# Seven products in place of eight for the second layer's up projection, in the last six pairs of token blocks

## What is computed

```python
def _moe2_ref(x, w_in, w_out, g_ln):        # x: 3072 x 512, w_in: 512 x 1024, w_out: 1024 x 512
    h = x @ w_in
    e = np.exp(h - np.max(h, axis=-1, keepdims=True))
    sm = e / (np.sum(e, axis=-1, keepdims=True) + 1e-09)
    solu = h * sm
    mu = np.mean(solu, axis=-1, keepdims=True)
    var = np.mean((solu - mu) ** 2, axis=-1, keepdims=True)
    ln = (solu - mu) / np.sqrt(var + 1e-06) * g_ln
    return (ln @ w_out).astype(np.float32)
```

## Time and profile before

| | us |
|---|---|
| median of 3 runs (lowest, highest) | 970.91 (968.33, 972.44) |
| the profiled execution's own time | 976.88 |
| its span from the first to the last instruction | 975.1 |
| TensorE matmuls busy | 944.7 (97%), 5334 matmuls |
| VectorE, ScalarE, GpSimd busy | 644.2 (66%), 521.7 (54%), 136.4 (14%) |
| mean granted TensorE clock | 0.989 |

### The profile page before, as it was taken

How to read it: one execution, slowest core, us unless ns; L and a number is a source line. 1 busy time by engine, 2 the same in 40 slices (tenths; PEclk the granted TensorE clock), 3 DMA queues, 4 the chain that set the end, 5 groups by cost and what they waited for, 6 DMA issues and landing times.

```text
span 975.1 us, 14652 instructions
## 1 busy us (share of the span) xinstructions
PE 944.7 (97%) x5334; PEld 834.8 (86%) x5334; DVE 644.2 (66%) x1065; ACT 521.7 (54%) x911; POOL 136.4 (14%) x170
## 2 busy tenths in 40 slices
PE   8979999999999999999999999999999999999996
PEld 4666787787899999999999999999888888888875
DVE  3677895786778754454679877777375766666651
ACT  3554644554556433342546554555477866666641
POOL 4313301101115430000053101010100000000000
PEclk9799999999999999999999999999999999999998
DMA  9656545626153423131364616340510054351533
GB/s 271 194 168 201 171 165 164 194 114 189 48 215 115 157 80 121 50 127 52 131 226 146 235 57 232 111 166 25 179 57 32 20 143 91 94 128 46 110 85 86
DMA packets 103847, 126.61 MB, mean 130 GB/s; under 512 B 8160, under 2 KB 84320, under 8 KB 103776
## 3 DMA queue, kind: packets, MB, share of 16 engines
q1 hardware_dynamic: 98320, 109.28, 36.5%
q0 software_dynamic: 4736, 15.73, 4.7%
q10 hardware_dynamic: 720, 0.66, 0.2%
HBM read 77.41 MB, written 37.75 MB: 118 GB/s over the span
## 4 chain that ended last, share of the span: by engine, by line
PE 81%; DVE 7%; DMA 3%; issue 3%; ACT 2%; SPq 2%; POOL 0%; DVEq 0%; ACTq 0%; POOLq 0%
PE psum L949 11%; PE psum L952 11%; PE psum L951 11%; PE psum L385 7%; PE psum L386 7%; PE psum L387 7%; PE psum L985 6%; PE psum L987 6%; PE psum L988 6%; PE psum L842 3%; PE psum L876 3%; PE psum L866 2%; PE psum L855 2%; SPq L690 1%; DMA out<-out_buf 1%
## 5 line engine op out<-in xcount | busy, mean ns | idle before, releaser
L949 PE MATMUL psum<-xo_hi,w_hi 128*128 128x384 f32 x560 | 194.8, 348 | 6.5 <-DVE psum L1658 2.5
L951 PE MATMUL psum<-xo_lo,w_hi 128*128 128x384 f32 x560 | 187.9, 336 | 0.0
L952 PE MATMUL psum<-xo_hi,w_lo 128*128 128x384 f32 x560 | 187.9, 336 | 0.0
L949 PEld LDWEIGHTS psum<-xo_hi,w_hi 128*128 128x128 f32 x560 | 105.7, 189 | 12.7 <-DVE c L1662 4.4
L951 PEld LDWEIGHTS psum<-xo_lo,w_hi 128*128 128x128 f32 x560 | 105.7, 189 | 0.8 <-issue 0.3
L952 PEld LDWEIGHTS psum<-xo_hi,w_lo 128*128 128x128 f32 x560 | 105.4, 188 | 0.0
L1163 ACT ACTIVATE xo_hi<-b 128x768 fp32r<-128x768 f32 x84 | 70.7, 846 | 63.2 <-PE psum L988 52.4
L1538 DVE TENSOR_TENSOR xo_lo<-b,xo_hi 128x768 fp32r<-128x768 f32 x84 | 81.3, 970 | 34.6 <-ACT xo_hi L1163 34.4
L385 PE MATMUL psum<-w_in_hi,x_hi 128*128 128x512 f32 x192 | 75.9, 395 | 2.0 <-ACT h_buf L1284 2.0
L1658 DVE TENSOR_TENSOR psum<-psum,p_buf 128x384 f32<-128x384 f32 x48 | 27.1, 565 | 76.0 <-PE psum L952 76.0
L385 PE MATMUL psum<-w_out_hi,ln_t_hi 128*128 128x512 f32 x192 | 75.1, 391 | 1.2 <-DVE ln_t_lo L1775 1.2
(11 more groups left out here) (142 smaller groups left out, 2030.2 us busy)
## 6 DMA issues: line engine op xcount, KB each, us to landing
act_dram<-act_buf SPq DMA_DIRECT2D x48, 384.0 KB, 2.4
b<-act_dram SPq DMA_DIRECT2D x48, 384.0 KB, 4.8
ln_t<-z SPq DMA_DIRECT2D x80, 128.0 KB, 3.1
kq_buf<-k_t SPq DMA_DIRECT2D x32, 192.0 KB, 2.7
kq_buf<-q_t SPq DMA_DIRECT2D x64, 96.0 KB, 3.0
q_dec<-q_t SPq DMA_DIRECT2D x32, 192.0 KB, 2.5
w_raw<-weights POOLq DMA_DIRECT2D x12, 512.0 KB, 5.1
x_dram<-x_tile SPq DMA_DIRECT2D x4, 1536.0 KB, 6.0
```

Of the source, the lines that this page charges most:

```text
L949: pe.matmul(dst, hi[:, cols], xo_hi[:, i, kc, :], start=i in (P1, P7) and kc == 0, stop=False, skip_group_check=True)
L951: pe.matmul(dst, hi[:, cols], xo_lo[:, i, kc, :], start=False, stop=False, skip_group_check=True)
L952: mm = pe.matmul(dst, lo[:, cols], xo_hi[:, i, kc, :], start=False, stop=kc == HK - 1, skip_group_check=True)
```

## The change

The up projection of pairs 6 to 11 (blocks 12 to 23) is computed by seven products. A pair is a 2 x 2 block problem: two blocks of tokens by two halves of the 512 input features, times two halves of the input features by two halves of the 1024 outputs. Each product is 2 chunks by 3 matmuls of 512 columns, so a pair has 42 matmuls for its up where it had 48. In the even step TensorE does P1, P7, P6, P2, P5 (30 matmuls) and then `down2`, in the odd step P3, P4 (12 matmuls) and then `down2`. Sums of products accumulate in PSUM with copies in between: ScalarE copies P1's bank into another (`copy_xy`) and P7 out (`copy_p7`), VectorE adds twice (`add_u3`, `add_c22`), ScalarE copies three of the four quarters out (`copy_up`).

The four sums of the weights (8 pieces of 128 x 512) are made by GpSimd in stage D at t = 1 between its stores, and each is stored to DRAM before the next is made. In stage C GpSimd loads them back, and ScalarE and VectorE split them (`t_high`, `t_low`): pieces 0 to 3 in tile 0, 4 to 7 in steps (1, 0) and (1, 1). The four sums of the tokens are made for each pair by GpSimd (`make_s`), and the seven operands of 2 x 128 columns are split in three instructions on each engine (`s_high`, `s_low`; 512, 256 and 1024 columns).

Memory: `z` has one buffer in place of two, `x2_raw` is loaded for one pair at a time (`load_up`), `squares` takes the place of `d_squares`.

The core of the diff: GpSimd's sums of weights, TensorE's products and their order, ScalarE's order in a pair of steps, the wait ahead of the transpose, VectorE's order.

```diff
+        UP_ORDER = (P1, P7, P6, P2, P5, P3, P4)
+            def sum_t(p, a, at):
...
+                    pool.wait_ge(t_summed, at)
+                    pool.wait_ge(t_stored, DMA * at)
+                pool.tensor_tensor(t_sum[:], first, second, ALU.subtract).then_inc(t_summed, 1)
+                pool.wait_ge(t_summed, at + 1)
+                pool.dma_start(t_store(T_PIECES.index((p, a))), t_sum[:]).then_inc(t_stored, DMA)
             for t in range(B):
+                sum_some(t, 0, 4)
                 for q in range(2):
                     store_x2(t, q, 0, q, c11_copied, q)
+                sum_some(t, 4, 6)
                 for q in range(2):
                     store_x2(t, 2 + q, 1, 2 + q, c22_summed, q)
+                sum_some(t, 6, 8)
...
+            def up_product(k, i):
+
+                if i in (P1, P2):
+                    pe.wait_ge(s_lo_ready, 3 * k + 1)
+                else:
+                    pe.wait_ge(s_lo_ready, 3 * k + 3)
...
+                elif i in (P6, P2):
+                    pe.wait_ge(up_xy_copied, k + 1)
+                elif i in (P5, P4):
+                    pe.wait_ge(up_u3_ready, k + 1)
+                else:
+                    pe.wait_ge(up_c22_ready, k + 1)
...
-                    if run_up_of(t, j):
-                        both_up(*run_up_of(t, j))
+                    if pair_up(t, j) is not None:
+                        for i in UP_ORDER[0:5] if j % 2 == 0 else UP_ORDER[5:7]:
+                            up_product(pair_up(t, j), i)
                     both_down2(t, j)
...
+                    k = pair_up(t, j)
+                    a, b = blocks_of(k)
+                    if j % 2 == 0:
+                        if j > 0:
+                            scale_out(t, j - 1)
+                        elif t > 1:
+                            scale_out(t - 1, 3)
+                        copy_xy(k)
+                        both_high(t, j)
+                        copy_p7(k)
+                        square_solu(*last_of(k))
+                        deviation_of_pair(last_of(k)[0], last_of(k)[1] // 2)
+                        copy_up(k, P2, UX, 0, 0, up_c11_copied)
+                        if k + 1 < PAIRS:
+                            s_high(k + 1, 0)
+                        continue
                     both_high(t, j)
+                    scale_out(t, j - 1)
+                    copy_up(k, P3, UY, 0, 1, up_c12_copied)
+                    copy_up(k, P4, UV, 1, 0, up_c21_copied)
+                    exponent(*a)
+                    if k + 1 < PAIRS:
+                        s_high(k + 1, 1)
+                        s_high(k + 1, 2)
+                    else:
                         both_high(*next_block(t, j))
+                    exponent(*b)
+                    square_solu(*a)
...
-                        at_least(dve, ln_t_moved[i], DMA * PARTS * (t - 2))
-                dve.transpose(z_of(t)[:, :, :, j, :].rearrange("p k f c -> p (k f) c"),
+                        at_least(dve, ln_t_moved[i], DMA * PARTS * (t - 1))
+                dve.transpose(z[:, :, :, j, :].rearrange("p k f c -> p (k f) c"),
...
                     both_low(t, j)
                     if j % 2 == 0:
+                        add_u3(k)
+                        invert_pair(last_of(k)[0], last_of(k)[1] // 2)
+                        add_c22(k)
+                        turn_up(last_of(k)[0], last_of(k)[1] - 1)
+                        turn_up(*last_of(k))
+                        if k + 1 < PAIRS:
+                            s_low(k + 1, 0)
+                        continue
+                    row_max_up(k, 0)
+                    row_max_up(k, 1)
+                    take_up(*a)
+                    if k + 1 < PAIRS:
+                        s_low(k + 1, 1)
+                        s_low(k + 1, 2)
+                    else:
                         both_low(*next_block(t, j))
+                    take_up(*b)
```

More of the change, by code:

```diff
@@ L709, in stage_c @@
                     store_out(0, 1)
+                    load_up(0)
                     store_out(0, 2)
@@ L712, in stage_c @@
                     return
-                if t + 2 < C_TILES:
-                    load_pair(t + 2)
-                store_out(t - 1, 3)
                 for j in range(3):
+                    if j % 2 == 0 and pair_up(t, j) is not None and pair_up(t, j) + 1 < PAIRS:
+                        load_up(pair_up(t, j) + 1)
+                    if j == 0:
+                        store_out(t - 1, 3)
                     if (t, j) == (C_TILES - 2, 2):
@@ L1325, in deviation_of_pair, with t_high, s_high, copy_xy @@
                                bias=eps_col[:], scale=1.0 / F2).then_inc(pair_std_ready, 1)
+            def t_high(i):
+                act.wait_ge(t_loaded[i % 2], DMA * (i // 2 + 1))
+                if T_PIECES[i][0] in (P6, P5):
+                    act.wait_ge(turned, 2 * BLOCKS)
+                elif T_PIECES[i][0] == P4:
+                    act.wait_ge(h_done, 4 * FIRST_PAIR)
+                act.activation(t_piece(i)[0], t_stage(i)[:], ACT.Copy).then_inc(t_hi_ready, 1)
+            def s_high(k, part):
+                raw = x2_raw[0]
+                if k == 0:
+                    act.wait_ge(h_done, 4 * FIRST_PAIR)
+                else:
+                    act.wait_ge(up_product_done, up_done(k - 1, P2 if part == 0 else P4))
+                if part < 2:
+                    act.wait_ge(x2_loaded[0], DMA * (4 + k))
+                    rows, src = ((slice(0, KC), raw[:, :, 0:P]), (slice(KC, KC + HK), raw[:, HK:KC, P:2 * P]))[part]
+                else:
+                    act.wait_ge(s_made, 4 * (k + 1))
+                    rows, src = slice(KC + HK, PRODUCTS * HK), s_raw[:]
+                act.activation(s_hi[:, rows, :], src, ACT.Copy).then_inc(s_hi_ready, 1)
+            def copy_xy(k):
+                act.wait_ge(up_product_done, up_done(k, P1))
+                at_least(act, up_c12_copied, k)
+                act.activation(psum[:, UY, :], psum[:, UX, :], ACT.Copy).then_inc(up_xy_copied, 1)
+            def copy_p7(k):
+                act.wait_ge(up_product_done, up_done(k, P7))
+                at_least(act, up_c22_ready, k)
+                act.activation(up_p7[:], psum[:, UV, :], ACT.Copy).then_inc(up_p7_copied, 1)
+            def copy_up(k, i, bank, which, s, copied):
+                t, j = blocks_of(k)[which]
+                act.wait_ge(up_product_done, up_done(k, i))
+                at_least(act, solu_ready, t * BLOCKS + j - 1)
+                act.activation(h_buf[:, j % 2, s * BANK:(s + 1) * BANK], psum[:, bank, :], ACT.Copy).then_inc(copied, 1)
             def deviation_of_one(j):
@@ L1400, in stage_c @@
                     x2_high(1, 1)
+                    for i in (0, 1):
+                        t_high(i)
                     take_up(1, 0)
@@ L1428, in stage_c @@
                     deviation(0, 3)
+                    for i in (2, 3):
+                        t_high(i)
                     exponent(2, 0)
@@ L1849, in stage_c @@
                     x2_low(1, 1)
+                    for i in (0, 1):
+                        t_low(i)
                     row_max(1, 0)
```

259 lines of the change are left out of this document (219 added, 40 removed).

## The result

The changed kernel took 974.87 us in the median of 10 runs (973.38 to 979.21), beside 970.64 us for 10 runs of the kernel before: a ratio of 1.0042, 95% interval 1.0029 to 1.0054. Forecast was 968.8. A second set of runs gave 1.0033 (1.0020 to 1.0045). So the change costs 3.5 to 4.2 us where it was to save 2.1.

The account below looks back on a forecast made before the run. TensorE's matmul count was taken to bound stage C's steps. Terms -6.80 + 2.1 + 0.5 + 1.8 + 0.3 + 0 = -2.1 us took the median from 970.91 to 968.8 us, 8-in-10 range 964.8 to 975.0.

Parts of the forecast that it names:

- ScalarE's ring: Stage C pair, ScalarE's work from P4's end to copy_xy: 8.13 us against 8.16 us of TensorE cover.
- What is removed: Stage C up products: 36 matmuls fewer, 8.16 us at most, 6.80 us sure from five pairs.
- The entry: Tile 2's first transpose waits for the single z's moves; TensorE stands still 2.1 us before (1, 1)'s down, bounds 0.6 and 4.
- The steady pair on ScalarE: Stage C pairs: ScalarE's work just fits its cover; 0.1 us stall for each of five pairs, bounds 0 and 0.6.
- rival (1): Stage C pairs: ScalarE's work exceeds its cover by 1.4 us, +6.5 us in sum, 975.3; chance 0.13.
- rival (3): Pairs starting at (2, 0) and (3, 0): x lands late behind the moves, 2 x 3 us, 974.8; chance 0.08.
- The steady pair on VectorE: Stage C pairs: the last s_low is done 6.65 us after P4's end, against 6.80 us of cover, so it fits.
- The end: Last pair: down (5, 0) starts 35.5 us after (4, 0) in place of 33.7, costing 1.8 us, bounds 0.8 and 3.
- The clock at the end: TensorE's two idle times before the downs of (4, 3) and (5, 0) may bring half clock: 0.3 us, bounds 0 and 1.3.
- Stage D: GpSimd's weight sums and stores delay nothing: cost 0, far bound 3 us; as a rival 971.8, chance 0.08.
- Rival (2): Entry and end of stage C cost little: -5.4 us, 965.5, to -8.2 if the sixth pair gives too; chance 0.14.
- (5): Stage C: the products do not shorten the step, as their matmuls cost more: 975; chance 0.01.

Follow-up runs that it names:

- before_again: The kernel before, unchanged, profiled a second time: 970.3 us, span 968.5.
- after_again: The changed kernel, unedited, in its second set of runs: ratio 1.0033 to the kernel before.
- pieces_after_moves: Changed kernel with three new orders, loads of pieces 4 and 5 held until tile 1's moves landed, splits of 4 to 7 later: 967.08 us, ratio 0.9956.
- last_pair_in_one_step: Changed kernel with the last pair's seven products all in step (4, 0), P4 before P3: 971.32 us, ratio 0.9998.
- pieces_later_alone: Changed kernel with only the splits of pieces 2 and 3 moved later in tile 0: 974.33 us, ratio 1.0033.

## Why the prediction was wrong, point by point

The median of 974.87 us is inside the stated range, 964.8 to 975.0, by 0.13 us, but the sum had the wrong sign: faster was forecast and slower came. That it stands in the range is luck. Its upper part was there for the rivals on ScalarE's ring, on stage D and on x: the first two did not come, and the third came with 0.9 us in place of 6.

Taken from the forecast's sum, against before_again in stage C: -2.1 us were forecast, +3.3 came, 5.4 us apart. 4.4 lie in the entry, 0.7 in the five pairs, 0.4 in the end.

**What is removed: right.** 5298 matmuls, and 20.40 us for a pair where nothing is late (803.17 to 823.57).

**The entry: the term that failed, 2.1 us forecast, 6.5 measured.** The wait was the one named: the first transpose of tile 2 waits for the moves, pieces and row maximum stand behind it, and `both_low` of (1, 1) comes late. The chain behind it was right too: from the transpose to TensorE 7.4 us were laid out (792.0 to 799.4), and 7.38 came (788.60 to 795.98). Two steps were off.
- *The landing of the moves.* In the forecast the last was issued 11.5 us after the first, as in the earlier trace rows, and landed 3.1 us later, the median of the earlier trace rows: 77.78 us after the first turn. It came at 80.44. The loads of pieces 4 and 5 were counted as splits on VectorE and nowhere as traffic. Leaving them out gives 78.11, 2.33 us less. The remaining 0.3 is a sum of two: the single `z` alone gave 77.11, 0.67 earlier than forecast, and without the loads the changed kernel is 1.00 later than that, 0.66 of it because its moves start later (63.83 us after the first turn, 63.17 with the single `z` alone). I had put the shifts of `t_high` and `t_low` at nothing, "because the moves' landing is set by the z of tile 1": but they delay that `z` as well, and moving two of them back gave 1.1 us in the trace (0.8 against after_again). They were to delay TensorE by up to 0.6 us ahead of the wait; the gap before the down of (1, 0) grew by 1.2, which is inside the 4.7 us by which the down of (1, 1) comes late.
- *The clock.* An idle time of 3.2 us, which the forecast did not have, was followed by half clock: 1.75 us. 2.1 + 2.66 + 1.75 = 6.5.

The far bound of this term was 4 us, for a landing of 5.2 us, the longest of the earlier trace rows; the longest with the loads was 6.5 us.

**The single `z` alone: a wait with almost no cost.** By the forecast's own chain the wait without the pieces costs 0.8 us: 2.4 against a slack of 1.6 (795.7 to 797.33). The moves landed 0.67 us earlier than laid out, which leaves 0.1, and 0.2 came; the whole time did not move (1.0005). It was the theory of the experiment, 3 to 5 us, that took the wait for the cause. The cost came from the wait together with what stood behind it and what ran beside it: with the row maximum ahead no idle time is left before the down of (1, 1), and without the traffic it is 1.11 us in place of 3.24.

**The steady pair on ScalarE: right, and rival (1) did not come.** The ring takes 7.84 us where 8.13 was laid out, and the conversions of 256 and 1024 columns 0.31 and 0.95 to the next start, where I took 0.3 and 1.0. The root and the exponential start 1.3 us after their table load (829.96 after 828.67, 820.24 after 818.94), and the shortest and the median of this trace's 41 loads are 1.29 us from their start to the next instruction. The Trainium skill ("ScalarE: Activation LUTs", What ACT_TABLE_LOAD costs) has a drain of about 1.38 us beside the load. It does not show here. Of the 1.16 us that the five pairs lost, 0.94 are in the two that start at (2, 0) and (3, 0).

**x comes late: rival (3), right in place, smaller in size.** In those two pairs the load of x stands behind the moves (SyncE, VectorE and ScalarE):

```profile
816.87 13.55 SPq L772 DMA_DIRECT2D ln_t<-z  x16
...
833.56 1.25 DVE L2031 STREAM_TRANSPOSE z<-solu 128x1024 f32<-128x1024 f32 x1 [1.46 <-DMA ln_t<-z]
...
835.46 0.63 ACT L1533 ACTIVATE s_hi<-x_raw 128x512 fp32r<-128x512 f32 x1 [4.71 <-DMA x_raw<-x_dram]
```

The forecast took 12.22 us for the issuing of the 16 moves, from before, and had the last of them landed 7.6 to 8.7 us into the pair and x there at 10.4. In the changed kernel the moves follow 0.1 us behind the issue of an output's store (3.3 us before) and their issuing takes 13.4 to 13.6 us in tiles 2 to 4 (11.1 to 11.7 before), so the transpose starts at 10.0 and x is there at 11.9, almost where 12 was given as harmless. That the store is the reason was not tested. The pairs lose 0.36 and 0.58 us in place of 3 (in after_again 0.11 and 1.34, the second behind 0.94 us of idle time). Which of the two waits sets it in the changed kernel no run separates. When x was taken ahead, the wait for `z` grew and the stalls with it, which points to the moves for those orders.

**The steady pair on VectorE: right.** The last `s_low` ends 6.72 us after P4's end (forecast 6.65); TensorE waited for it 0.9 us in four weight loads together.

**The end: right for (5, 0).** 35.61 us against 35.5. The clock at the end (0.3) did not fall, after idle times of 1.75 and 1.40 us in a row. The other 0.6 us of the end lie behind (5, 0), most of them in an idle time of 0.70 us at 959.25 that ends with ScalarE's copy of an output (the largest gap of before_again behind (5, 0) is some 0.3 us over the usual distance); they were not in the sum.

**Stage D: right at 0.** GpSimd's sums took 1.3 to 2.0 us each, with the stores of x behind them, and TensorE's stage is as long as before, 174.7 us. The whole kernel's medians differ by 3.5 and 4.2 us and stage C by 3.3 and 3.5, so up to a microsecond outside what the traces compare is not excluded.

**The rivals on the whole.** The side above 975.8 had 0.10 and was built on the ring of ScalarE, which had been laid out instruction by instruction. The place that was not laid out, what else is on the DMA engines while the moves run, had a bound of 4 us and no rival of its own. Rival (2), entry and end at little cost, is what pieces_after_moves reaches: 88.99 us at the entry, 55.97 at the end, 4.1 us less in stage C than before. Two sums of the rivals were off by a little: (2) left out the 0.5 us of the ring (965.5 should be 966.0), and (5) gives 975.6, not 975.

## What to carry to other kernels

When a buffer goes from two to one, the wait that it adds is not the price: price what is queued behind the waiting instruction, and put there nothing that the next stage is waiting for. The row maximum, with the two low parts before it, moved ahead of the waiting transpose gave 4.8 us by the medians (974.87 to 970.12) with the transpose as late as before.

A prefetch that is "free" on every engine still travels. Put the transfers of a change on the same time axis as the transfers whose landing somebody waits for: two loads of 256 KB beside 16 moves made the waiting transpose 2.3 us later, and through a stall and the clock that was 3 to 4 us of the kernel.

Take a second profile before the terms are placed, if the first stands far off the median: here the stages ahead of the change differed by 6 us between two profiles of one kernel.

## What the runs showed of the hardware

- Idle times and the granted clock: idle times of 2.96 (after_again), 3.06 (last_pair_in_one_step), 3.24 (changed kernel) and 3.33 us (pieces_later_alone) were each followed by matmuls at half clock; in the changed kernel that cost 1.75 us. Idle times of 1.11, 1.47, 1.50, 1.71, and 1.75 followed seven us later by 1.40, were not. In the first profile of before one of 1.82 us was (a granted clock of 0.50 from 708 to 709 us), with a gap of 0.58 us from start to start 4.8 us ahead of it. These rows alone do not tell what decides between the two.
- 16 moves of 128 KB from SyncE's queue, from the first issue to the instruction that waits for the last landing: 13.9 to 14.4 us in four profiles without GpSimd's loads of 256 KB among them, 16.0 to 17.4 us in eight with them. In tile 1 their issuing took 11.1 to 12.2 us, with or without the loads, and 13.3 to 13.7 us in tiles 2 to 4 of the changed kernels (without x taken ahead), right behind a store's issue.
